# Attention, two expert layers and an ELU layer on one core: steps 0 and 1 of the experts interleaved with the attention's rounds

## What is computed

```python
# attention: batch 4, heads 8, seq 576, head_dim 64, chunks of 64 tokens
scores = scale * q_c @ k_c.T                     # 64 x 64 for each chunk and head
attn = exp(scores - max) ; attn /= attn.sum(-1) + 1e-9
x = (attn @ v_c) as [2304 tokens, 512]
# experts: 8, hidden 1024
P = exp(x @ w_gate - max) ; 8 times: rows /= sum + 1e-9, columns /= sum + 1e-9, P *= N / E
x2 = sum over e of P[:, e] * (relu(x @ w1[e]) @ w2[e])
# last layer, hidden 2048
h = x2 @ w_in ; out = elu(h) @ w_out             # output [2304, 512]
```

## Time and profile before

| | us |
|---|---|
| median of three runs | 1996.7 (1993.1 to 1996.8) |
| the profiled execution | 1995.5 |
| its span, first to last instruction | 1993.7 |
| TensorE busy | 1945.5 (98%) |
| VectorE busy | 1123.3 (56%) |
| ScalarE busy | 719.5 (36%) |
| GpSimd busy | 532.8 (27%) |

### The profile page before, as it was taken

The page is one execution under the profiler, slowest core; times in us unless marked ns, Lnnn a source line. Parts: engine busy times, 40 slices in busy tenths (PEclk is TensorE's granted clock), DMA queues, the critical chain, the costliest instruction groups (busy, mean ns, idle before and its releaser), DMA issues.

```text
span 1993.7 us, 31492 instructions
## 1 busy us (share of the span) xinstructions
PE 1945.5 (98%) x10738; PEld 1751.2 (88%) x10738; DVE 1123.3 (56%) x1866; ACT 719.5 (36%) x1516; POOL 532.8 (27%) x600
## 2 busy tenths in 40 slices
PE   6799999999999999999999999999999989999999
PEld 5699999988999889998899988999889868998888
DVE  7766654555545555455554555555555576666666
ACT  4532223222233323232223322223323455555554
POOL 5732252222222222222222222222222342222220
PEclk9999999999999999999999999999999989999999
DMA  8110000000000000000000000000000000000002
GB/s 257 52 39 26 22 21 22 21 21 21 21 21 21 21 21 32 31 21 21 21 21 21 21 21 21 21 21 21 21 25 28 11 21 22 21 21 21 21 21 95
DMA packets 20154, 61.40 MB, mean 31 GB/s; under 512 B 2960, under 2 KB 2960, under 8 KB 20112
## 3 DMA queue, kind: packets, MB, share of 16 engines
q1 hardware_dynamic: 20112, 60.84, 9.0%
HBM read 56.12 MB, written 4.72 MB: 31 GB/s over the span
## 4 chain that ended last, share of the span: by engine, by line
PE 93%; DVE 4%; ACT 1%; issue 0%; POOL 0%; ACTq 0%
PE bank L477 44%; PE bank L507 5%; PE bank L494 5%; PE bank L495 5%; PE bank L509 5%; PE bank L508 5%; PE bank L499 5%; PE last_banks L507 3%; PE last_banks L509 3%; PE last_banks L508 3%; PE last_banks L494 3%; PE last_banks L495 3%; PE last_banks L499 3%; DVE x_sum L991 1%; ACT x_hi L720 1%
## 5 line engine op out<-in xcount | busy, mean ns | idle before, releaser
L477 PE MATMUL bank<-x_hi,w_hi 128*128 128x384 f32 x1680 | 568.5, 338 | 14.5 <-DVE x_lo L1002 6.9
L477 PE MATMUL bank<-x_hi,w_lo 128*128 128x384 f32 x1680 | 565.9, 337 | 0.0
L477 PE MATMUL bank<-x_lo,w_hi 128*128 128x384 f32 x1680 | 564.6, 336 | 0.0
L746 ACT ACTIVATE h_raw<-bank 128x384 f32<-128x384 f32 x360 | 176.6, 491 | 746.5 <-PE bank L477 744.7
L1009 DVE TENSOR_TENSOR h_raw<-bank,h_raw 128x384 f32<-128x384 f32 x360 | 200.7, 558 | 421.2 <-PE bank L477 419.6
L477 PEld LDWEIGHTS bank<-x_hi,w_hi 128*128 128x128 f32 x1680 | 316.6, 188 | 24.9 <-issue 7.8
L477 PEld LDWEIGHTS bank<-x_lo,w_hi 128*128 128x128 f32 x1680 | 316.6, 188 | 5.5
L319 POOL TENSOR_TENSOR w_sum<-raw 128x256 f32<-128x256 f32 x40 | 29.5, 739 | 1088.6 <-PE bank L477 1081.7
L477 PEld LDWEIGHTS bank<-x_hi,w_lo 128*128 128x128 f32 x1680 | 316.4, 188 | 0.0
L1027 DVE SCALAR_TENSOR_TENSOR acc<-bank,route,acc 128x512 f32<-128x512 f32 x336 | 240.4, 751 | 125.4 <-PE bank L509 125.4
L755 ACT ACTIVATE h_hi<-h_raw 128x384 fp32r<-128x384 f32 x288 | 151.2, 526 | 208.6 <-DVE h_raw L1009 208.6
(11 more groups left out here) (103 smaller groups left out, 2561.0 us busy)
## 6 DMA issues: line engine op xcount, KB each, us to landing
raw<-in_w_up SPq DMA_DIRECT2D x40, 512.0 KB, 3.2
raw<-in_w_down SPq DMA_DIRECT2D x40, 512.0 KB, 3.3
qk<-in_q_k SPq DMA_DIRECT2D x18, 512.0 KB, 5.9
v_wide<-in_v SPq DMA_DIRECT2D x36, 128.0 KB, 3.6
out<-acc SPq DMA_DIRECT2D x18, 256.0 KB, 2.0
gate_w<-in_w_gate SPq DMA_DIRECT2D x1, 16.0 KB, 7.1
```

The lines of the kernel that those rows point to most:

```text
L477: mm = nc.tensor.matmul(up_ps[s], w[:, s, kk, :], xs[:, s, kk, :], start=first and s in (M1, M2, M5), stop=kk == 1 and w is w1_lo, skip_gr ...
L746: nc.scalar.activation(h_raw[:, to[0], to[1], :], src, ACT.Copy).then_inc(fork_done, 1)
```

## The change

- The attention has nine rounds ahead of step 0 (EARLY). Rounds 9 to 14 stand one before each product of step 0 (M1, M2, M5, M6, M3, M7: scores(i), turn(i-3), product, values(i-3)), rounds 15 to 20 in step 1 before M2 to M4. Steps 0 and 1 take the products in the order of the kind "first".
- In the early rounds scores alternate between two pairs of banks.
- v is loaded once, by one DMA into 128 partitions; values are 64-row matmuls, with no zeros; `zero` is gone.
- `soft` has a 65th column that holds 1e-9, so row_sum includes it and row_den is gone. norm writes to its own three buffers `prob`.
- The loads of qk and v are issued in another order, the first weights earlier.
- x_split(u, s) waits for each product's own x_lo, in all six steps with new x.
- Gates one pair later (0 and 1 in step 1, 2 and 3 behind it, 4 and 5 in step 2 after M7), balancing from step 4 on, `w1_sums(1)` ahead of the all-reduce, `scale_acc` in one block behind the fourth convert, gate constants on GpSimd behind norm(14).

The diff, cut to its core:

```diff
-TURN_LAG, VALUE_LAG = 3, 4
-
-OVERLAP = {M1: 18, M5: 19, M3: 20, M7: 21}
-FIRST_OVERLAP = 18
-
-LOWS_POOL = [7, 14, 17, 22, 27, 32]
-LOWS_DVE = [0, 0, 4, 6, 8, 10]
+TURN_LAG = 3
+EARLY = 9
+ROUND_OF = {0: {M1: 9, M2: 10, M5: 11, M6: 12, M3: 13, M7: 14}, 1: {M2: 15, M5: 16, M6: 17, M3: 18, M7: 19, M4: 20}}
+
+
+
+SUM_ORDER = [[M5, M6, M3, M7]] * 3 + [[M5, M6, M7, M3]] * 3
+X_ORDER = [PRODUCTS["first"], PRODUCTS["first"], PRODUCTS["relu"]] + [[M1, M2, M4, M5, M7, M6, M3]] * 3
+LOWS_POOL = [PRODUCTS["first"], PRODUCTS["first"], [M1, M5, M2, M4]] + [[M1, M2, M4, M5, M7]] * 3
+LOWS_DVE = [[], [], [M6, M3, M7]] + [[M6, M3]] * 3
...
-                for g in range(2):
-                    half = slice(CHUNK * g, CHUNK * g + CHUNK)
-                    sp.dma_start(v_wide[j][half, g, :, :, :], v[t, half, :, :, :]).then_inc(v_loaded[j], 16)
+                sp.dma_start(v_rows[j][:, :, :, :], v[t, :, :, :, :]).then_inc(v_loaded[j], 16)
 
             load_qk(0)
             load_qk(1)
+            sp.dma_start(raw1[:, :, :], w_up[0, :, :, :]).then_inc(raw1_loaded, 16)
+            load_qk(2)
             load_v(0)
-            load_qk(2)
+            load_qk(3)
             load_v(1)
-            load_qk(3)
+            sp.dma_start(raw2[:, :, :], w_down[0, :, :, :]).then_inc(raw2_loaded, 16)
             load_v(2)
             load_v(3)
-            for i in range(TILES):
-                if i + DEPTH < TILES:
-                    load_qk(i + DEPTH)
-                if DEPTH <= i:
-                    load_v(i)
-                if i == 1:
+            for i in range(DEPTH, TILES):
+                load_qk(i)
+                load_v(i)
+                if i == 8:
...
+            for j in range(3):
+                nc.gpsimd.memset(soft[j][:, :, HD:HD + 1], EPS).then_inc(eps_set, 1)
+            w1_sums(0)
...
+            norm(7)
+            x_low(0, M2)
+            norm(8)
+            norm(9)
+            x_low(0, M5)
...
+            w1_sums(1, 2, "relu")
             pool.wait_ge(part_max_done, 1)
             nc.gpsimd.partition_all_reduce(all_max, part_max, P, bass.bass_isa.ReduceOp.max).then_inc(all_max_done, 1)
-            for g in range(GPE):
-                if g == GPE - 1:
-                    pool.wait_ge(balance, BAL * SINKHORN_STEPS + 1)
-                    scale_acc(0)
+            w1_lows(1)
+            w2_lows(1)
+            for g in range(1, GPE):
                 convert(g + 1, PAIRS * g + 2, "relu")
-            scale_acc(1)
-            scale_acc(2)
+            pool.wait_ge(balance, BAL * SINKHORN_STEPS + 1)
+            for p in range(PAIRS):
+                scale_acc(p)
...
                 pe.wait_ge(qk_loaded[j], 16 * (i // DEPTH + 1))
-                if i >= 1:
+                if i >= EARLY:
                     pe.wait_ge(soft_done, i)
+                elif i >= 2:
+                    pe.wait_ge(soft_done, i - 1)
...
+                            cs, rows = slice(CHUNK * c, CHUNK * c + CHUNK), slice(HD * g, HD * g + HD)
+                            mm = nc.tensor.matmul(x_ps[i % 2][rows, m, cs], v_rows[j][rows, m, c, :], e_t[rows, m, cs],
+                                                  start=True, stop=True)
...
-            def x_split(u):
-                pe.wait_ge(x_lo_done, LOWS_POOL[u])
-                if LOWS_DVE[u] > 0:
-                    pe.wait_ge(x_lo_rest, LOWS_DVE[u])
-
-            def step(n, g, p, kind="relu", begin=False, x_ready=None, after=None, before_close=None):
+            def x_split(u, s):
+                if s in LOWS_POOL[u]:
+                    pe.wait_ge(x_lo_done, low_count(LOWS_POOL, u, s))
+                else:
+                    pe.wait_ge(x_lo_rest, low_count(LOWS_DVE, u, s))
...
+            for i in range(EARLY):
+                scores_of(i)
+                if i >= TURN_LAG:
                     turn_prob(i - TURN_LAG)
-                if i >= VALUE_LAG:
-                    values_of(i - VALUE_LAG)
-
-            for i in range(FIRST_OVERLAP):
-                attention(i)
-            step(0, 0, 0, begin=True, x_ready=0, after=overlap)
-            pe.wait_ge(const_ready, 2)
-            gate_of(0)
-            gate_of(1)
-
-            def gates_1(s):
+                if i > TURN_LAG:
+                    values_of(i - TURN_LAG - 1)
...
+            def round_begin(n):
+
+                def ahead(s):
+                    i = ROUND_OF[n].get(s)
+                    if i is None:
+                        return
+                    if i < TILES:
+                        if n == 1:
+                            pe.wait_ge(acc_done, 5)
+                        scores_of(i)
+                    if i == EARLY:
+                        values_of(i - TURN_LAG - 1)
+                    turn_prob(i - TURN_LAG)
+                return ahead
+
+            def round_end(n):
+                def after(s):
+                    i = ROUND_OF[n].get(s)
+                    if i is not None:
+                        if n == 1:
+                            pe.wait_ge(acc_done, 6)
+                        values_of(i - TURN_LAG)
+                    if n == 1 and s == M3:
+                        pe.wait_ge(const_ready, 2)
+                        gate_of(0)
+                        gate_of(1)
+                    if n == 1 and s == M4:
+                        gate_turn(0)
+                        gate_turn(1)
+                return after
...
-                nc.vector.tensor_scalar(row_den[:, :], row_sum[:, :], EPS, None, ALU.add).then_inc(sum_done, 1)
-                dve.wait_ge(sum_done, 3 * i + 2)
```

More of the change, by code:

```diff
@@ L78, in nth_hidden, with low_count @@
     return HIDDEN[kind].index(h) + 1
+def low_count(lows, u, s):
+    return sum(len(lows[v]) for v in range(u)) + lows[u].index(s) + 1
 def pair_tile(p, i):
@@ L864, in _ @@
-            relu_step(0, begin=True, after=overlap)
-            for c in range(3, 7):
-                x_high(0, 1, c)
-            for c in range(3):
-                x_high(0, 2, c)
+                    x_high(0, M2)
+            x_copy(5)
+            e_copy(6)
+            exp_of(9)
+            fork(0, up_a, H11, M1, "first")
+            x_copy(6)
+            e_copy(7)
+            x_high(0, M5)
+            exp_of(10)
+            x_copy(7)
+            x_high(0, M6)
+            e_copy(8)
@@ new lines, in _ @@
+            for i in range(1, EARLY):
+                softmax_head(i)
+                softmax_tail(i - 1)
+            softmax_head(9)
+            x_sums(0, (M5, M6))
+            softmax_tail(8)
+            softmax_head(10)
+            softmax_tail(9)
+            x_sums(0, (M3,))
+            softmax_head(11)
+            softmax_tail(10)
+            x_sums(0, (M7,))
+            softmax_head(12)
+            softmax_tail(11)
+            join(0, H11, up_c, M2, 1, "first")
+            softmax_head(13)
@@ new lines, in _ @@
+            softmax_tail(12)
+            low(0, H11, "first")
+            softmax_head(14)
+            softmax_tail(13)
+            join(0, H12, up_b, M3, 3, "first")
+            join(0, H22, up_a, M7, 2, "first")
+            low(0, H12, "first")
+            low(0, H22, "first")
+            low(0, H21, "first")
+            softmax_tail(14)
+            x_sums(1, (M5,))
+            for i in range(TPB):
+                add_tile(0, 0, i, "first")
+            x_sums(1, (M6,))
+            for i in range(TPB, 2 * TPB):
+                add_tile(0, 0, i, "first")
@@ new lines, in _ @@
+            x_sums(1, (M3,))
+            softmax_head(15)
+            x_sums(1, (M7,))
+            softmax_head(16)
+            softmax_tail(15)
+            join(1, H11, up_c, M2, 1, "first")
+            softmax_head(17)
+            softmax_tail(16)
+            low(1, H11, "first")
+            softmax_tail(17)
+            join(1, H12, up_b, M3, 3, "first")
+            join(1, H22, up_a, M7, 2, "first")
+            low(1, H12, "first")
+            low(1, H22, "first")
+            logits_of(0)
@@ L1153, in _ @@
-            relu_step(1, 1, "first", after=logits_1)
-            def logits_2(where):
-                if where == "begin":
+                if where == "low21":
                     logits_of(4)
```

492 lines of the change are left out of this document (263 added, 229 removed).

## The result

| | before | after |
|---|---|---|
| median, us | 1995.5 (1993.1 to 1996.8, 4 runs) | 2018.4 (2017.2 to 2019.9, 4 runs) |
| ratio after to before | | 1.0116, 95% interval 1.0099 to 1.0134 |
| profiled execution, us | 1995.5 | 2017.2 |
| its span, us | 1993.7 | 2015.3 |
| TensorE busy, us | 1945.5 | 1950.8 |

The change makes the kernel slower by 23 us, that is 1.2%. The forecast had 2000.2 and a range of 1986 to 2011: it was 18 us too low, and the range did not reach the result. That it said slower is worth little, since its +3.5 lay within the 4 us that it called hard to tell from no change. The last two rows of the table say where to look: 22.6 us are lost ahead of step 3, and the part behind it gains 1.0 us. So the change does start its products 10.6 us earlier, and has lost all of that and 22.6 more some 100 us later.

The account below looks back on a forecast made before the run. The prediction took the attention at the head as the bound, with a loop on SyncE's queue: step 3 starts 7.8 us later, less 4.4 gained at 1627, +3.5 as rounded, on the median 1996.7 gives 2000.2 us; 8 in 10: 1986 to 2011.

Parts of the forecast that it names:

- scores of 9 start: Attention on TensorE: scores of round 9 start at 56.3 us, after rounds of 7.8 us from round 5 on.
- step 0 ends: End of the first step of products, with attention rounds 9 to 14 in it: 95.5 us, before 98.1.
- step 1, with gates 0 and 1: Second step of products, with attention rounds 15 to 20 and a gate pair: from 95.5 to 125.1 us.
- gates 2 and 3, step 2: A gate pair of 2.8 us, then step 2 with another pair and two transposes, 19.3 us: ends at 147.2.
- wait ahead of step 3: New wait of TensorE for the first low part of the next weights, behind GpSimd's all-reduce: 1.9 us.
- gain behind it: Finer waits for x_lo near 1627 us, at step 97: gain 4.4 us, bounds 3 and 6.9.
- The loop on SyncE's queue: Attention rounds 5 to 9: v waits for values four rounds back, the next round's qk stands behind it; 7.8 us a round.
- Rival 2: The loop on SyncE's queue does not bind, only the loads do: scores of 9 at 31, 1967 us; chance 0.05.
- The price of 64-row values: TensorE in the attention: values cost what scores do, 1.1 us at 1.2 GHz or 0.65 at 2.4; bounds 1.9 or 1.1.
- The all-reduce: GpSimd ahead of step 3: held 7.2 us from 140.7, to 147.9, with the next weights' low parts queued behind.
- The finer waits: Step 97: M1, M2 and M5 run from 1620.5 us, M6 at 1625.0, M3 at 1627.4; gain 4.4 us.
- Rival 3: GpSimd's norm and x_lo bound steps 0 and 1: 0.8 us in each of eleven rounds, +9, 2009 us; chance 0.23.

Follow-up runs that it names:

- the first experiment: The changed kernel with the order of loads on SyncE's queue put back to that of before, qk(i+4) ahead of v(i): 1989.6 us, 0.997 of before.

## Why the prediction was wrong

By its own marks (all in us; the last column is what the step added to the error):

| step | forecast | measured | error |
|---|---|---|---|
| scores of 9 start | 56.3 | 57.56 | +1.3 |
| step 0 ends | 95.5 | 97.85 | +1.1 |
| step 1, with gates 0 and 1 | 29.6 | 34.2 | +4.6 |
| gates 2 and 3, step 2 | 22.1 | 22.9 | +0.8 |
| wait ahead of step 3 | 1.9 | 9.04 | +7.1 |
| gain behind it | -4.4 | -1.0 | +3.4 |

Together 18.3, the whole distance between 2000.2 and 2018.4. The start of the scores of 9 hides three errors: those of 4 start at 16.1 and not at 17.3, the four rounds to those of 8 take 1.1 longer, and the last takes 9.2 instead of 7.8, with `gate_w` loaded ahead of qk(9), a term that the forecast did not have.

**The loop on SyncE's queue: right**, in mechanism, place and nearly in size; the size by luck in part, as the next paragraph says. Rival 2, that it does not bind, is what the first experiment made true: scores of 9 at 30.3 (it had 31), but M4 of step 0 starting at 62 where it had M4 over at 56, since GpSimd's x_lo cost 6.7 us that its rounds of 3.5 did not hold.

**The price of 64-row values: mis-sized**, and two errors hid each other in the loop. I took the price of scores, 1.1 or 0.65, and had the right one, 1.9 or 1.1, only as the other bound. It cost 0.85 in each round at 1.2 GHz and 0.5 in each later one. The landing went the other way: from issue of v to scores it took 3.95 us (20.19 to 24.14) and not 4.5. So 8.07 came out against 7.8. My value was the middle of the bounds, and the upper one came from a qk behind two halves of v; one v is not two. The estimate of 3.8 from the Trainium skill, "DMA: Bandwidth & Descriptors", section "Anatomy of one DMA", agrees with the 3.95 of the trace to 0.15 us, and was nearer than mine. In step 1 nothing made up for the dearer values: six of them are 3.0 of its 4.6, and a wait of 0.75 for the copy of e_t is in no step of the forecast. That I chose the end from "also 32 matmuls on 64 rows" was the fault: the row of scores shows a price for four quarters, and the diff says that values write to two.

**The all-reduce: the step that failed most.** "7.2 us, though only 0.38 is shown as busy" was read from the earlier trace rows as the length of the all-reduce. It is the way back alone. The way in was in the same row, hidden in "22.10 <-DVE" (as the kernel with the all-reduce ahead of the sums shows for this order), and the change takes that cover away by putting the sums, which wait for a DMA until 147.22, ahead of it. I called the moved sums "hidden ahead of the reduce" and did not ask what they hid. They also ended 1.8 us behind the maximum of the logits (150.17 against 148.39), with which the forecast began the all-reduce. So the first low part came at 163.16: the 13.0 us behind the last sum are 5.8 more than my 7.2, and with the 1.8, less the 0.4 that I had added for M5 and that did not come, they are the 7.1 of the table to 0.1.

**The finer waits: the first half right, the second wrong.** M1 to M5 run at once and M6 waits, as told. "What is late next" named the join of H11 only for the downs. ScalarE's queue has the negation of H11 ahead of the fork of H22, so the same join holds up M3 as well. With the forks first, 0.9 us of waiting come back by the rows and 1.9 us by the medians; the rest stays with the join and with x_lo.

**Rival 3**, slower by GpSimd's norm and x_lo, came true as a mechanism and not as a price. In steps 0 and 1 TensorE waits 4.4 us for x_lo, all of it in step 0 and most of it ahead of M5, M7 and M4, and 2.3 us for qk. But the forecast had GpSimd's pair in its rounds already, and from the scores of 9 to its end step 0 took only 1.1 us more than forecast, where rival 3 had 0.8 in each round with a product.

What stays open: why step 1 has some 0.6 us more than the values, the copy of e_t and the later qk explain, and why the clock in the head differs between kernels whose edits all lie behind it (0.75 to 0.83 up to 61 us in the profiles with the loop). The 65th column and the missing row_den were not tried by themselves.

## What to carry to other kernels

In an in-order queue of loads, write each entry with what it waits for and when that comes; a load needed in the next round behind one that waits for this round makes a loop of the load's whole latency; the four buffers of this kernel did not help. When an instruction is moved, look at what its old wait was covering, not only at how long it is shown busy: an idle time put down to a releaser may hold another cost that shows once the releaser is early. And where a row is taken as the price of a new form of matmul, compare which parts of the array the two use, not only their shapes.

## What the runs showed of the hardware

- GpSimd took 5.59 to 6.73 us ahead of an all-reduce over the partitions and 6.65 to 7.25 us ahead of the next tensor_tensor, each time and not once; a memset between them did not wait. At the head, with the first loads in flight, the way in took 10.46 us.
- 32 products of 64 rows and 64 columns took 1.13 us at 1.2 GHz and 0.69 us at 2.4 GHz in four quarters of the array, and 1.98 and 1.15 us in two, the same as the old values with zeros in half of 128 rows. Leaving out the zeros gained TensorE nothing.
- The granted clock follows the gaps: between 36 and 65 us, in the loop, it is 0.61 on average where it was 1.00 before, and 0.74 between 155 and 175 us, where the gap of 9.04 us lies. A wait thus costs more than its length here: behind the 4.24 us ahead of M3 the products take 0.52 us (granted clock 0.53 from 1654 to 1660) where they took 0.34 ahead of it.
